# Attention value products in three 256-column chunks, two of them issued inside their own head

## The chip, the cores and the metric

The program runs on one core of a Trainium2 chip. The metric is the device time of one execution in microseconds (us), the median of the runs; lower is better.

## What is computed

The input holds queries, keys and values of 2 x 8 = 16 heads (here "heads" counts both batches), 768 rows of 64 channels each. Rows attend only inside their cluster; two mixture-of-experts layers follow, which the change doesn't touch.

```python
q_assign = argmax(einsum(q_n, c_n)); k_assign = argmax(einsum(k_n, c_n))
mask = q_assign[:, :, :, None] == k_assign[:, :, None, :]
scores = np.where(mask, scale * q @ k.T, -1e9)
attn = np.exp(scores - scores.max(-1)); attn /= attn.sum(-1) + 1e-9
return attn @ v                      # then _moe_ref and _moe2_ref
```

## The kernel before

All of the attention is one software pipeline over 16 heads `n`, each of six steps `t` of 128 query rows. The four compute engines and the DMA queue of SyncE (SP) each have their own program, written out by hand in `pair`, with counting semaphores between them; an engine works strictly in its own order. `j` is the parity of the head, `g = 6n + t`.

One step of 128 rows passes through these functions:

- **score** (TensorE, L1063 and L1064): two products of 512 and two of 256 columns into one of two score buffers. It is issued one step ahead.
- **row_top** (VectorE, L906): the maximum of the 768 scores of each row.
- **exp** (ScalarE, L731): the exponential, with the row's sum.
- **turn_probs** (TensorE, L1072): six 128x128 transposes, in two halves of three, into two PSUM banks (4 and 5). It is issued one step late.
- **high** (ScalarE, L714) copies the two halves, rounded to fp32r, into `p_hi`; **low** (VectorE, L912) writes the remainders into `p_lo`. The next `turn_probs` needs `low` of the same half.
- **sum_values** (TensorE, L1090 and L1091): the value product. For each of six key blocks it multiplies `v_both` (values, and their remainders in the other 64 columns) with `p_hi` and with `p_lo`, summed in the PSUM region `side` (banks 6 and 7). Part 0 and part 1 hold six products of 512 columns each, part 2 twelve of 256 columns.
- **o_copy** (ScalarE, L708) copies the sums to `o_sb`, first 512 columns, then 256. **fold_output** (TensorE, L1102, six matmuls recorded as twelve rows) turns them into rows and adds the two parts; **store_head** (VectorE, L932, L939, L946) scales and stores them.

For the head to come, TensorE computes cluster scores (**cluster_scores**, L1040), VectorE picks the cluster in five steps (**choose**, L881 to L897), TensorE turns the one-hot rows (**turn_onehot**, L1050), and ScalarE copies them into mask rows (**mask_rows**, L697 and L699). GpSimd splits queries and keys of a head (**split_qk**, L262 to L268) and its values (**split_v**, L596 and L599); SP loads them (**load_qk**, L473; **load_v**, L478).

TensorE's order in head `n` at each step is: score of `t+1`, turn_probs of `t-1`, and then

- t = 0: cluster scores of head n+1; t = 1: fold_output of head n-2; t = 2: turn_onehot of head n+1;
- t = 3, 4, 5: sum_values parts 0, 1, 2 of head **n-1**.

Part 0 waits until the mask rows are copied, since `side` overlaps the bank of the turned one-hot rows. ScalarE's order is: exp of `t`, high of `t-1`, and at t = 2 then mask_rows, at t = 5 then o_copy of the first 512 columns; the other 256 are copied at t = 0 of the next head. VectorE has store_head of head n-2 at t = 3. After the last head TensorE still has turn_probs, parts 0 and 1 of head 15, fold_output of head 14, part 2 and fold_output of head 15. `p_hi` and `p_lo` hold a whole head each, two buffers of each.

Of the kernel before, what the change touches and what calls it, by code (L numbers as in the profile page):

```python
# [14 lines left out]
F32 = mybir.dt.float32  # L15
# [7 lines left out]
P = 128  # L23
# [20 lines left out]
QK_SPLITS = 5  # L44
WIDE = DM + 2
# [13 lines left out]
def build(nc, q, k, v, centroids, w_gate, w_noise, noise, w1, w2, w_gate2, w1b, w2b, capacity, out):  # L59
# [6 lines left out]
    with ExitStack() as ctx:  # L66
# [14 lines left out]
        p_hi = [carve(QT * S).rearrange("p (k q) -> p k q", k=QT) for _ in range(2)]  # L81
        p_lo = [carve(QT * S).rearrange("p (k q) -> p k q", k=QT) for _ in range(2)]
# [88 lines left out]
        side = bank(6, 1024)  # L171
        o_sum = bank(7, QT * FOLD).rearrange("p (t d) -> p t d", t=QT)
        HALVES = ((0, 3), (3, 6))

        def turned_half(c):
            return bank(4 + c, 3 * P)

# [283 lines left out]
        def _(sp):  # L461
# [41 lines left out]
            with sp.Fori(1, HEADS // 2) as r:  # L503
                for j in range(2):
                    load_qk(2 * r + j, j)
                    load_v(2 * r + j - 1, 1 - j)

                blank(rows[0], TILES * DM, 4 * DM, r - 1)
# [44 lines left out]
        def _(gp):  # L553
# [37 lines left out]
            def split_v(m, j, r):  # L591

                gp.wait_ge(values_landed[j], 16 * (r + 1))
                need(gp, values_summed, 2 * (m - 1))
                gp.sem_inc(passed, 1)
                gp.tensor_copy(v_both[j][:, :, 0:D], v_raw[j]).then_inc(v_split, 1)  # L596
                gp.wait_ge(v_split, 2 * m + 1)
                gp.sem_inc(passed, 1)
                gp.tensor_tensor(v_both[j][:, :, D:P], v_raw[j], v_both[j].bitcast(F32)[:, :, 0:D],  # L599
                                 ALU.subtract).then_inc(v_split, 1)  # L600
# [86 lines left out]
        def _(act):  # L687
# [14 lines left out]
            def o_copy(n, part):  # L702

                act.wait_ge(values_summed, 2 * n + 1 + part)
                if part == 0:
                    need(act, o_folded, n)
                lo, hi = ((0, 512), (512, S))[part]
                act.activation(o_sb[:, lo:hi], side[:, lo:hi], ACT.Copy).then_inc(o_copied, 1)  # L708

            def high(g, j, t):  # L710

                for c, (a, b) in enumerate(HALVES):
                    act.wait_ge(probs_turned, 2 * g + c + 1)
                    act.activation(p_hi[j][:, a:b, t * P:(t + 1) * P],  # L714
                                   turned_half(c).rearrange("p (k q) -> p k q", k=3), ACT.Copy).then_inc(high_ready, 1)
# [4 lines left out]
            def pair(i, first=False, last=False):  # L720
                for j in range(2):
                    n = 2 * i + j
                    prepares = not (last and j == 1)
                    follows = not (first and j == 0)
                    for t in range(QT):
                        g = QT * n + t
                        act.wait_ge(top_ready, g + 1)
                        need(act, probs_turned, 2 * (g - 1))
                        if t == 0:
                            need(act, inv_step, 2 * (n - 1))  # L730
                        act.activation(probs[t % 2], scores[t % 2], ACT.Exp, bias=top[:, t % 2:t % 2 + 1],  # L731
                                       accum_out=sums[:, j, t:t + 1]).then_inc(probs_ready, 1)
                        if t == 0 and not first:
                            o_copy(n - 2, 1)
                        if t > 0:
                            if t == 1:
                                need(act, values_summed, 2 * (n - 1))
                            high(g - 1, j, t - 1)
                        elif follows:
                            high(g - 1, 1 - j, QT - 1)  # L740
                        if t == 2 and prepares:
                            mask_rows(n + 1, 1 - j, False)
                            mask_rows(n + 1, 1 - j, True)
                        if t == 5 and follows:
                            o_copy(n - 1, 0)
# [5 lines left out]
            high(QT * HEADS - 1, 1, QT - 1)  # L751
            o_copy(HEADS - 2, 1)
            o_copy(HEADS - 1, 0)
            o_copy(HEADS - 1, 1)

# [88 lines left out]
        def _(dve):  # L844
# [63 lines left out]
            def low(g, j, t, c):  # L908

                a, b = HALVES[c]  # L910
                dve.wait_ge(high_ready, 2 * g + c + 1)
                dve.tensor_tensor(p_lo[j][:, a:b, t * P:(t + 1) * P],  # L912
                                  turned_half(c).rearrange("p (k q) -> p k q", k=3),
                                  p_hi[j][:, a:b, t * P:(t + 1) * P].bitcast(F32), ALU.subtract).then_inc(low_ready, 1)
# [44 lines left out]
            def pair(i, first=False, last=False):  # L959
                for j in range(2):  # L960
# [3 lines left out]
                    for t in range(QT):  # L964
                        g = QT * n + t

                        def store_all():
                            if isinstance(i, int):
                                b, h = (n - 2) // H, (n - 2) % H
                            else:  # L970
                                b, h = bass.ds((i - 1) // 4, 1), bass.ds(2 * ((i - 1) % 4) + j, 1)
                            for step in range(3):
                                store_head(n - 2, j, b, h, step)
# [24 lines left out]
            dve.wait_ge(const_ready, 23)  # L998
# [7 lines left out]
            for j in range(2):  # L1006
                for step in range(3):
                    store_head(HEADS - 2 + j, j, B - 1, H - 2 + j, step)
# [20 lines left out]
        def _(pe):  # L1029
# [4 lines left out]
            def cluster_scores(m, j, r, h):  # L1034
# [3 lines left out]
                need(pe, o_copied, 2 * m - 5)  # L1038
# [37 lines left out]
            def sum_values(n, j, part, prepares=False):  # L1076


                if part == 0:
                    pe.wait_ge(low_ready, 2 * (QT * n + 4))  # L1080
                    pe.wait_ge(v_split, 2 * (n + 1))
                    need(pe, o_copied, 2 * n - 1)
                    if prepares:
                        pe.wait_ge(rows_ready, 2 * n + 6)
                if part == 2:
                    pe.wait_ge(low_ready, 2 * QT * (n + 1))
                    need(pe, head_stored, n)
                a, b = (512, S) if part == 2 else (0, 512)
                for kb in range(QT) if part == 2 else range(*HALVES[part]):
                    pe.matmul(side[:, a:b], v_both[j][:, kb, :], p_hi[j][:, kb, a:b], start=(kb == 0), stop=False)  # L1090
                    mm = pe.matmul(side[:, a:b], v_both[j][:, kb, :], p_lo[j][:, kb, a:b], start=False,  # L1091
                                   stop=(kb == QT - 1))
                if part:
                    mm.then_inc(values_summed, 1)

            def fold_output(n, h):


                pe.wait_ge(o_copied, 2 * n + 2)
                need(pe, head_stored, n)  # L1100
                for t in range(QT):
                    mm = pe.matmul(bank(7, 512)[:, t * FOLD:(t + 1) * FOLD + GROUP], o_sb[:, t * P:(t + 1) * P],  # L1102
# [8 lines left out]
            def pair(i, first=False, last=False):  # L1111
                for j in range(2):
# [3 lines left out]
                    for t in range(QT):  # L1116
# [12 lines left out]
                        if t == 1 and not first:  # L1129
                            fold_output(n - 2, 2 * ((i - 1) % 4) + j)  # L1130
                        if t >= 3 and follows:
                            sum_values(n - 1, 1 - j, t - 3, prepares)
                        if t == 2 and prepares:
                            turn_onehot(n + 1, 1 - j)

            pair(0, first=True)
            pe.wait_ge(const_ready, 23)
            pe.wait_ge(fold_landed, 64)
# [127 lines left out]
```

## Time and profile before

| | |
|---|---|
| median of 3 timed runs | 1020.16 us (1014.76, 1020.16 and 1021.29) |
| span of the profiled execution, first to last instruction | 1015.0 us |
| its own time beyond the span | not given |
| TensorE busy | 865.7 us (85%) |
| VectorE, ScalarE, GpSimd busy | 569.2, 349.7, 542.1 us |
| mean granted TensorE clock | 0.915 |

The profile is one execution. Each row names an engine (PE is TensorE's matmuls, PEld its weight loads, DVE VectorE, ACT ScalarE, POOL GpSimd), a source line and an operation. Attention takes the first 291 us or so. Ends of matmuls are modelled, so positions on TensorE are best read from starts.

### The profile page before, as it was taken

To read this page: it belongs to the slowest core of one execution; us is meant where nothing else is said; L and a number is where in the kernel's file an instruction comes from. 1 tells how busy PE (TensorE), PEld (TensorE's weight loads), DVE (VectorE), ACT (ScalarE), POOL (GpSimd) and SP (SyncE) were. 2 spreads that over 40 slices of the span, in tenths; PEclk is the share of its full clock that TensorE was granted. 3 is DMA by queue.
4 is the path that set the end of the run, shared out by engine and by line. 5 is a ranking of instruction groups with operands and counts; after the bars stand their busy time and mean duration, and the time that the engine had idled before them with its cause. 6 is when DMAs were issued, how large, how long until landed. Compare 5 with 4: busy or idle time off the path is not lost.

```text
span 1015.0 us, 16573 instructions
## 1 busy us (share of the span) xinstructions
PE 865.7 (85%) x4669; PEld 734.4 (72%) x4670; DVE 569.2 (56%) x907; ACT 349.7 (34%) x586; POOL 542.1 (53%) x338
## 2 busy tenths in 40 slices
PE   4899999999932199999999999999493099999995
PEld 3788888888832078888878887878393078888884
DVE  6888888888851044444444444444273436665552
ACT  3878787877840121131112212020000212343210
POOL 6666665657134863364334615160362926798563
PEclk9999999999975599999999999999755589999998
DMA  7544345346643653354334525251262624566422
GB/s 162 151 122 125 88 116 142 104 109 252 254 147 142 217 188 124 124 171 159 124 124 145 176 74 171 76 175 52 85 184 84 217 80 166 193 241 209 156 103 93
DMA packets 70742, 147.83 MB, mean 146 GB/s; under 512 B 23296, under 2 KB 23296, under 8 KB 68416
## 3 DMA queue, kind: packets, MB, share of 16 engines
q1 hardware_dynamic: 38096, 60.77, 19.8%
q10 hardware_dynamic: 26624, 67.12, 19.8%
q0 software_dynamic: 6000, 19.68, 5.7%
q8 instruction: 10, 0.16, 0.1%
q14 instruction: 12, 0.10, 0.0%
HBM read 107.66 MB, written 39.88 MB: 145 GB/s over the span
## 4 chain that ended last, share of the span: by engine, by line
PE 72%; issue 8%; POOL 7%; DVE 5%; DMA 3%; ACT 2%; SPq 1%; ACTq 0%; POOLq 0%; DVEq 0%
PE banks L1209 15%; PE banks L1211 15%; PE banks L1210 15%; PE banks L1072 5%; PE banks L1090 4%; POOL rows_by_slot L664 3%; PE banks L1091 3%; PE banks L1224 3%; PE banks L1063 3%; PE banks L1064 3%; PE banks L1040 2%; PE banks L1102 2%; PE banks L1200 2%; DMA tokens_and_shared<-rows_by_slot 2%; POOL tokens_and_shared L278 2%
## 5 line engine op out<-in xcount | busy, mean ns | idle before, releaser
L648 POOL TENSOR_TENSOR arena<-raw_ring,arena 128x1024 fp32r<-128x1024 f32 x128 | 302.3, 2399 | 262.5 <-ACT arena L786 262.1
L786 ACT ACTIVATE arena<-raw_ring 128x1024 fp32r<-128x1024 f32 x128 | 133.2, 1058 | 460.2 <-PE banks L1211 278.0
L1209 PE MATMUL banks<-arena,split_x 128*128 x352 | 143.0, 406 | 16.1 <-DVE split_x L416 14.4
L1209 PE MATMUL banks<-arena,split_h 128*128 x352 | 142.4, 405 | 7.5 <-DVE split_h L444 5.9
L1211 PE MATMUL banks<-arena,split_x 128*128 x352 | 139.8, 397 | 0.0
L1210 PE MATMUL banks<-arena,split_x 128*128 x352 | 139.5, 396 | 0.0
L1211 PE MATMUL banks<-arena,split_h 128*128 x352 | 138.6, 394 | 0.0
L1210 PE MATMUL banks<-arena,split_h 128*128 x352 | 138.4, 393 | 0.0
L422 DVE TENSOR_SCALAR tokens_and_shared<-banks 128x512 f32<-128x512 f32 x88 | 60.8, 690 | 104.5 <-PE banks L1211 104.0
L912 DVE TENSOR_TENSOR arena<-banks,arena 128x384 fp32r<-128x384 f32 x192 | 99.0, 542 | 19.5 <-ACT arena L714 19.5
L906 DVE TENSOR_REDUCE top<-banks 128x1 f32<-128x768 f32 x96 | 91.1, 949 | 21.4 <-PE banks L1064 20.6
L714 ACT ACTIVATE arena<-banks 128x384 fp32r<-128x384 f32 x192 | 85.0, 489 | 40.7 <-PE banks L1072 39.1
L731 ACT ACTIVATE tokens_and_shared<-banks,top 128x768 f32<-128x768 f32 x96 | 86.9, 905 | 15.2 <-DVE top L906 14.8
L1209 PEld LDWEIGHTS banks<-arena,split_x 128*128 128x128 f32 x352 | 67.4, 191 | 30.5 <-issue 17.4
L429 DVE COPY tokens_and_shared<-banks 128x512 f32<-128x512 f32 x29 | 20.1, 692 | 123.1 <-PE banks L1211 123.1
L1072 PE MATMUL banks<-ident,tokens_and_shared 128*128 128x128 f32 x576 | 84.9, 279 | 4.2 <-DVE arena L912 3.9
L1200 PE MATMUL banks<-ident,tokens_and_shared 128*128 128x128 f32 x184 | 28.7, 280 | 67.7 <-DMA tokens_and_shared<-rows_by_slot 67.7
L1209 PEld LDWEIGHTS banks<-arena,split_h 128*128 128x128 f32 x352 | 67.0, 190 | 21.5 <-issue 9.1
L1211 PEld LDWEIGHTS banks<-arena,split_x 128*128 128x128 f32 x352 | 67.2, 191 | 14.4
L1211 PEld LDWEIGHTS banks<-arena,split_h 128*128 128x128 f32 x352 | 66.9, 190 | 14.2
L1200 PEld LDWEIGHTS banks<-ident,tokens_and_shared 128*128 128x128 f32 x184 | 23.1, 143 | 74.7 <-DMA tokens_and_shared<-rows_by_slot 69.1
L1210 PEld LDWEIGHTS banks<-arena,split_x 128*128 128x128 f32 x352 | 67.5, 192 | 13.2
(161 smaller groups left out, 1466.9 us busy)
## 6 DMA issues: line engine op xcount, KB each, us to landing
raw_ring<-in_moe_w ACTq DMA_DIRECT2D x128, 512.0 KB, 3.4
rows_by_slot<-arena SPq DMA_DIRECT2D x8, 1024.0 KB, 6.0
raw_ring<-in_q SPq DMA_DIRECT2D x40, 192.0 KB, 3.5
raw_ring<-in_k SPq DMA_DIRECT2D x40, 192.0 KB, 4.0
tokens_and_shared<-rows_by_slot SPq DMA_DIRECT2D x30, 256.0 KB, 3.3
results_by_slot<-tokens_and_shared SPq DMA_DIRECT2D x29, 256.0 KB, 2.1
rows_by_slot<-arena SPq DMA_DIRECT2D x5, 1028.0 KB, 10.4
tokens_and_shared<-rows_by_slot SPq DMA_DIRECT2D x16, 257.0 KB, 3.7
```

The costliest lines, as they stand in the source:

```text
L422: dve.tensor_scalar(h_tile[:, half * 512:(half + 1) * 512], bank(2 + half, 512), 0.0, None, ALU.max).then_inc(z.relu_done, 1)
L648: gp.tensor_tensor(arena[:, lo:lo + PIECE], ring[:, slot * PIECE:(slot + 1) * PIECE], arena[:, hi:hi + PIECE].bitcast(F32), ALU.subtract). ...
L714: act.activation(p_hi[j][:, a:b, t * P:(t + 1) * P], turned_half(c).rearrange("p (k q) -> p k q", k=3), ACT.Copy).then_inc(high_ready, 1)
L731: act.activation(probs[t % 2], scores[t % 2], ACT.Exp, bias=top[:, t % 2:t % 2 + 1], accum_out=sums[:, j, t:t + 1]).then_inc(probs_ready, 1)
L786: act.activation(arena[:, hi:hi + PIECE], ring[:, slot * PIECE:(slot + 1) * PIECE], ACT.Copy).then_inc(w_high, 1)
L906: dve.tensor_reduce(top[:, b:b + 1], scores[b], AX, ALU.max, negate=True).then_inc(top_ready, 1)
L912: dve.tensor_tensor(p_lo[j][:, a:b, t * P:(t + 1) * P], turned_half(c).rearrange("p (k q) -> p k q", k=3), p_hi[j][:, a:b, t * P:(t + 1) * ...
L1072: mm = pe.transpose(turned_half(c)[:, (k - a) * P:(k - a + 1) * P], probs[t % 2][:, k * P:(k + 1) * P], ident[:, :])
L1200: mm = pe.transpose(bank(0, DM)[:, b * P:(b + 1) * P], x_tile[:, b * P:(b + 1) * P], ident[:, :])
L1209: pe.matmul(out_ap, left[:, 0, tile], hi, start=(b == 0), stop=False)
L1210: pe.matmul(out_ap, left[:, 0, tile], lo, start=False, stop=False)
L1211: mm = pe.matmul(out_ap, left[:, 1, tile], hi, start=False, stop=(b == blocks - 1))
```

## The change

`sum_values` now has three equal chunks of 256 columns, each of twelve products with its own sum in one PSUM region `summed` of 256 columns (bank 7). Chunks 0 and 1 of head n are issued in head n itself, at t = 4 and t = 5, chunk 2 at t = 1 of head n+1. fold_output moves to t = 3 and to head n-1, writes into bank 6 and waits for the mask rows; store_head moves to t = 4 and to head n-1. ScalarE copies chunk 0 at t = 5 after `high`, chunk 1 at t = 0 of the next head after `high`, chunk 2 at t = 2 before `mask_rows`. `p_hi` and `p_lo` shrink to two chunks each. GpSimd and SP take a head's values ahead of the next head's queries and keys. After the last head only chunk 2 and one fold_output are left.

```diff
-        p_hi = [carve(QT * S).rearrange("p (k q) -> p k q", k=QT) for _ in range(2)]
+        p_hi = [carve(QT * CHUNK).rearrange("p (k q) -> p k q", k=QT) for _ in range(2)]
...
-        side = bank(6, 1024)
-        o_sum = bank(7, QT * FOLD).rearrange("p (t d) -> p t d", t=QT)
+        summed = bank(7, CHUNK)
+        o_sum = bank(6, QT * FOLD).rearrange("p (t d) -> p t d", t=QT)
...
+            return (CHUNKS * j + t // 2) % 2, slice(t % 2 * P, (t % 2 + 1) * P)
...
+                    load_v(2 * r + j - 1, 1 - j)
                     load_qk(2 * r + j, j)
-                    load_v(2 * r + j - 1, 1 - j)
...
-                need(gp, values_summed, 2 * (m - 1))
+                need(gp, values_summed, CHUNKS * (m - 1))
...
+            split_v(0, 0, 0)
             split_qk(1, 1, 0)
-            split_v(0, 0, 0)
             with gp.Fori(1, HEADS // 2) as r:
+                split_v(2 * r - 1, 1, r - 1)
                 split_qk(2 * r, 0, r)
-                split_v(2 * r - 1, 1, r - 1)
+                split_v(2 * r, 0, r)
                 split_qk(2 * r + 1, 1, r)
-                split_v(2 * r, 0, r)
...
+            def high(g, n, j, t):
+
+                buf, at_q = chunk_place(j, t)
+                if t % 2 == 0:
+                    need(act, values_summed, CHUNKS * n + t // 2 - 1)
...
-                        if t == 0 and not first:
-                            o_copy(n - 2, 1)
                         if t > 0:
-                            if t == 1:
-                                need(act, values_summed, 2 * (n - 1))
-                            high(g - 1, j, t - 1)
+                            high(g - 1, n, j, t - 1)
                         elif follows:
-                            high(g - 1, 1 - j, QT - 1)
+                            high(g - 1, n - 1, 1 - j, QT - 1)
+                            o_copy(n - 1, 1)
+                        if t == 2 and follows:
+                            o_copy(n - 1, 2)
                         if t == 2 and prepares:
                             mask_rows(n + 1, 1 - j, False)
                             mask_rows(n + 1, 1 - j, True)
-                        if t == 5 and follows:
-                            o_copy(n - 1, 0)
+                        if t == 5:
+                            o_copy(n, 0)
...
-                            if t == 3 and not first and place == 2:
+                            if t == 4 and follows and place == 2:
...
+            def sum_values(n, j, chunk):
+
+
+                pe.wait_ge(low_ready, 2 * (QT * n + 2 * chunk + 2))
+                if chunk == 0:
                     pe.wait_ge(v_split, 2 * (n + 1))
...
+                need(pe, o_copied, CHUNKS * n + chunk)
+                buf = (CHUNKS * j + chunk) % 2
+                for kb in range(QT):
+                    pe.matmul(summed, v_both[j][:, kb, :], p_hi[buf][:, kb, :], start=(kb == 0), stop=False)
+                    mm = pe.matmul(summed, v_both[j][:, kb, :], p_lo[buf][:, kb, :], start=False,
                                    stop=(kb == QT - 1))
...
+                mm.then_inc(values_summed, 1)
+
+            def fold_output(n, h, turned):
+
+
+                pe.wait_ge(o_copied, CHUNKS * (n + 1))
+                pe.wait_ge(rows_ready, 2 * turned)
...
-                        if t == 1 and not first:
-                            fold_output(n - 2, 2 * ((i - 1) % 4) + j)
-                        if t >= 3 and follows:
-                            sum_values(n - 1, 1 - j, t - 3, prepares)
+                        if t == 1 and follows:
+                            sum_values(n - 1, 1 - j, 2)
                         if t == 2 and prepares:
                             turn_onehot(n + 1, 1 - j)
+                        if t == 3 and follows:
...
+                            fold_output(n - 1, 2 * ((i + j - 1) % 4) + 1 - j, n + 1 + prepares)
+                        if t >= 4:
+                            sum_values(n, j, t - 4)
...
             turn_probs(QT * HEADS - 1, QT - 1)
-            sum_values(HEADS - 1, 1, 0)
-            sum_values(HEADS - 1, 1, 1)
-            fold_output(HEADS - 2, H - 2)
             sum_values(HEADS - 1, 1, 2)
-            fold_output(HEADS - 1, H - 1)
+            fold_output(HEADS - 1, H - 1, HEADS)
```

## Rows read from the trace of the kernel before

**Rows 1.** Windows: each engine's busy time, clock, DMA share, GB/s, by stretch.

```profile
100.00:150.00 50.00, 49.72 (x347) 43.61 (x347) 43.14 (x86) 39.74 (x86) 31.79 (x22) 1.00 0.40 104
```

**Rows 2.** Waits between 50 and 250 us: total us, times, longest.

```profile
POOL arena L262 <- PE banks L1064: 64.2, 12, 5.4
...
PEld banks L1072 <- DVE arena L912: 4.2, 27, 0.2
PEld banks L1090 <- ACT arena L699: 3.9, 12, 0.4
```

**Rows 3.** Timeline of PE, head 5: start, duration, engine, line, operation.

```profile
104.07 0.82 PE L1072 MATMUL banks<-ident,tokens_and_shared 128*128 128x128 f32 x6
104.73 1.49 PE L1102 MATMUL banks<-fold_all,tokens_and_shared 128*128 x12
105.99 0.47 PE L1063 MATMUL banks<-arena 128*128 128x512 f32 x1
...
106.78 0.82 PE L1072 MATMUL banks<-ident,tokens_and_shared 128*128 128x128 f32 x6
...
109.88 0.50 PE L1090 MATMUL banks<-arena 128*128 128x512 f32 x1
...
111.37 0.40 PE L1063 MATMUL banks<-arena 128*128 128x512 f32 x1
...
112.08 0.82 PE L1072 MATMUL banks<-ident,tokens_and_shared 128*128 128x128 f32 x6
112.65 0.48 PE L1090 MATMUL banks<-arena 128*128 128x512 f32 x1
...
114.11 0.39 PE L1063 MATMUL banks<-arena 128*128 128x512 f32 x1
...
114.93 1.01 PE L1072 MATMUL banks<-ident,tokens_and_shared 128*128 128x128 f32 x6
115.70 0.36 PE L1090 MATMUL banks<-arena 128*128 128x256 f32 x1
...
117.20 0.40 PE L1063 MATMUL banks<-arena 128*128 128x512 f32 x1
```

**Rows 4.** Timeline of ACT in the same head.

```profile
107.31 0.87 ACT L714 ACTIVATE arena<-banks 128x384 fp32r<-128x384 f32 x2 [0.88 <-PE banks L1072]
108.20 0.80 ACT L697 ACTIVATE arena<-banks 16x768 fp32r<-16x768 bf16 x1
```

**Rows 5.** Lines by form, 50 to 250 us: busy, mean ns, idle before.

```profile
L714 ACT ACTIVATE arena<-banks 128x384 fp32r<-128x384 f32 x145 | 64.2, 489 | 27.5 <-PE banks L1072 26.1
...
L708 ACT ACTIVATE tokens_and_shared<-banks 128x256 f32<-128x256 f32 x12 | 4.7, 395 | 0.0
```

**Rows 6.** Timeline of PE: a step of heads 0, 1 and 14.

```profile
30.56 0.48 PE L1063 MATMUL banks<-arena 128*128 128x512 f32 x1
...
39.33 1.18 PE L1072 MATMUL banks<-ident,tokens_and_shared 128*128 128x128 f32 x6 [1.53 <-DVE arena L912]
...
255.93 0.82 PE L1072 MATMUL banks<-ident,tokens_and_shared 128*128 128x128 f32 x6
```

**Rows 7.** Windows in head 1, columns as in rows 1.

```profile
40.00:42.00 2.00, 2.00 (x11) 1.57 (x12) 1.97 (x4) 1.54 (x3) 0.99 (x1) 0.61 0.45 121
```

**Rows 8.** Timeline of PE in head 15 and after it.

```profile
268.78 0.98 PE L1072 MATMUL banks<-ident,tokens_and_shared 128*128 128x128 f32 x6 [0.41 <-DVE arena L912]
...
280.39 0.82 PE L1072 MATMUL banks<-ident,tokens_and_shared 128*128 128x128 f32 x6
...
286.26 0.36 PE L1090 MATMUL banks<-arena 128*128 128x256 f32 x1 [0.96 <-DVE tokens_and_shared L939]
...
288.41 1.59 PE L1102 MATMUL banks<-fold_all,tokens_and_shared 128*128 128x112 f32 x12 [0.47 <-ACT tokens_and_shared L708]
```

**Rows 9.** Timeline of DVE: the last `low`.

```profile
282.01 0.52 DVE L912 TENSOR_TENSOR arena<-banks,arena 128x384 fp32r<-128x384 f32 x1
```

**Rows 10.** Windows after the last head, columns as in rows 1.

```profile
284.00:286.00 2.00, 1.30 (x12) 1.12 (x11) 0.60 (x2) 0.60 (x1) 0.00 (x0) 1.00 0.00 0
```

More of the change, by code:

```diff
@@ L44 @@
 QK_SPLITS = 5
+CHUNK = 2 * P
+CHUNKS = S // CHUNK
 WIDE = DM + 2
@@ L79, in carve @@
             return arena[:, at[0] - size:at[0]]
-        p_hi = [carve(QT * S).rearrange("p (k q) -> p k q", k=QT) for _ in range(2)]
-        p_lo = [carve(QT * S).rearrange("p (k q) -> p k q", k=QT) for _ in range(2)]
+        p_hi = [carve(QT * CHUNK).rearrange("p (k q) -> p k q", k=QT) for _ in range(2)]
+        p_lo = [carve(QT * CHUNK).rearrange("p (k q) -> p k q", k=QT) for _ in range(2)]
         q_both, k_high, q_mask, k_mask = ([carve(S) for _ in range(2)] for _ in range(4))
@@ L176, in turned_half, with chunk_place @@
             return bank(4 + c, 3 * P)
+        def chunk_place(j, t):
+            return (CHUNKS * j + t // 2) % 2, slice(t % 2 * P, (t % 2 + 1) * P)
         passed = sem("passed")
@@ L700, in mask_rows, with o_copy @@
                                    scale=FAR, bias=-FAR).then_inc(rows_ready, 1)
-            def o_copy(n, part):
-                act.wait_ge(values_summed, 2 * n + 1 + part)
-                if part == 0:
+            def o_copy(n, chunk):
+                act.wait_ge(values_summed, CHUNKS * n + chunk + 1)
+                if chunk == 0:
                     need(act, o_folded, n)
-                lo, hi = ((0, 512), (512, S))[part]
-                act.activation(o_sb[:, lo:hi], side[:, lo:hi], ACT.Copy).then_inc(o_copied, 1)
-            def high(g, j, t):
+                act.activation(o_sb[:, chunk * CHUNK:(chunk + 1) * CHUNK], summed, ACT.Copy).then_inc(o_copied, 1)
+            def high(g, n, j, t):
+                buf, at_q = chunk_place(j, t)
+                if t % 2 == 0:
+                    need(act, values_summed, CHUNKS * n + t // 2 - 1)
                 for c, (a, b) in enumerate(HALVES):
                     act.wait_ge(probs_turned, 2 * g + c + 1)
-                    act.activation(p_hi[j][:, a:b, t * P:(t + 1) * P],
+                    act.activation(p_hi[buf][:, a:b, at_q],
                                    turned_half(c).rearrange("p (k q) -> p k q", k=3), ACT.Copy).then_inc(high_ready, 1)
@@ L750, in _ @@
             pair(HEADS // 2 - 1, last=True)
-            high(QT * HEADS - 1, 1, QT - 1)
-            o_copy(HEADS - 2, 1)
-            o_copy(HEADS - 1, 0)
+            high(QT * HEADS - 1, HEADS - 1, 1, QT - 1)
             o_copy(HEADS - 1, 1)
+            o_copy(HEADS - 1, 2)
             weights = ((w1, w2), (w1b, w2b))
@@ L910, in low @@
                 a, b = HALVES[c]
+                buf, at_q = chunk_place(j, t)
                 dve.wait_ge(high_ready, 2 * g + c + 1)
-                dve.tensor_tensor(p_lo[j][:, a:b, t * P:(t + 1) * P],
+                dve.tensor_tensor(p_lo[buf][:, a:b, at_q],
                                   turned_half(c).rearrange("p (k q) -> p k q", k=3),
-                                  p_hi[j][:, a:b, t * P:(t + 1) * P].bitcast(F32), ALU.subtract).then_inc(low_ready, 1)
+                                  p_hi[buf][:, a:b, at_q].bitcast(F32), ALU.subtract).then_inc(low_ready, 1)
             def invert(n, j, step):
@@ L968, in store_all @@
                             if isinstance(i, int):
-                                b, h = (n - 2) // H, (n - 2) % H
+                                b, h = (n - 1) // H, (n - 1) % H
                             else:
-                                b, h = bass.ds((i - 1) // 4, 1), bass.ds(2 * ((i - 1) % 4) + j, 1)
+                                b, h = bass.ds((i + j - 1) // 4, 1), bass.ds(2 * ((i + j - 1) % 4) + 1 - j, 1)
                             for step in range(3):
-                                store_head(n - 2, j, b, h, step)
+                                store_head(n - 1, 1 - j, b, h, step)
                         def between(place):
@@ L983, in between @@
                                 choose(n + 1, 1 - j, 2 + place)
-                            if t == 3 and not first and place == 2:
+                            if t == 4 and follows and place == 2:
+                                if first:
+                                    dve.wait_ge(const_ready, 23)
                                 store_all()
@@ L997, in _ @@
             pair(0, first=True)
-            dve.wait_ge(const_ready, 23)
             with dve.Fori(1, HEADS // 2 - 1) as i:
@@ L1005, in _ @@
             low(QT * HEADS - 1, 1, QT - 1, 1)
-            for j in range(2):
-                for step in range(3):
-                    store_head(HEADS - 2 + j, j, B - 1, H - 2 + j, step)
+            for step in range(3):
+                store_head(HEADS - 1, 1, B - 1, H - 1, step)
             for s in range(2):
@@ L1037, in cluster_scores @@
                 pe.wait_ge(head_landed[j], 16 * 6 * (r + 1))
-                need(pe, o_copied, 2 * m - 5)
+                need(pe, head_stored, m - 2)
                 for t in range(QT):
@@ L1074, in turn_probs @@
                     mm.then_inc(probs_turned, 1)
-            def sum_values(n, j, part, prepares=False):
-                if part == 0:
-                    pe.wait_ge(low_ready, 2 * (QT * n + 4))
+            def sum_values(n, j, chunk):
+                pe.wait_ge(low_ready, 2 * (QT * n + 2 * chunk + 2))
+                if chunk == 0:
                     pe.wait_ge(v_split, 2 * (n + 1))
[L1082 to L1091, printed above, removed]
-                                   stop=(kb == QT - 1))
[L1093 to L1100, printed above, removed]
+                need(pe, o_copied, CHUNKS * n + chunk)
[3 more added lines that the diff above has]
+                    mm = pe.matmul(summed, v_both[j][:, kb, :], p_lo[buf][:, kb, :], start=False,
+                                   stop=(kb == QT - 1))
+                mm.then_inc(values_summed, 1)
+            def fold_output(n, h, turned):
+                pe.wait_ge(o_copied, CHUNKS * (n + 1))
+                pe.wait_ge(rows_ready, 2 * turned)
                 for t in range(QT):
-                    mm = pe.matmul(bank(7, 512)[:, t * FOLD:(t + 1) * FOLD + GROUP], o_sb[:, t * P:(t + 1) * P],
+                    mm = pe.matmul(bank(6, 512)[:, t * FOLD:(t + 1) * FOLD + GROUP], o_sb[:, t * P:(t + 1) * P],
                                    fold_all[:, bass.ds(h * FOLD, FOLD + GROUP)], start=True, stop=True)
@@ L1128, in pair @@
                             cluster_scores(n + 1, 1 - j, i + j, 2 * ((i + j) % 4) + 1 - j)
-                        if t == 1 and not first:
-                            fold_output(n - 2, 2 * ((i - 1) % 4) + j)
-                        if t >= 3 and follows:
-                            sum_values(n - 1, 1 - j, t - 3, prepares)
+                        if t == 1 and follows:
+                            sum_values(n - 1, 1 - j, 2)
                         if t == 2 and prepares:
                             turn_onehot(n + 1, 1 - j)
+                        if t == 3 and follows:
+                            if first:
+                                pe.wait_ge(const_ready, 23)
+                                pe.wait_ge(fold_landed, 64)
+                            fold_output(n - 1, 2 * ((i + j - 1) % 4) + 1 - j, n + 1 + prepares)
+                        if t >= 4:
+                            sum_values(n, j, t - 4)
             pair(0, first=True)
-            pe.wait_ge(const_ready, 23)
-            pe.wait_ge(fold_landed, 64)
             with pe.Fori(1, HEADS // 2 - 1) as i:
```

## The prediction

> **What bounds the kernel now.** The page's busy times name TensorE first, but over stages with different limits, so I read the windows next. In the attention TensorE's matmuls fill 49.72 of 50 us at full clock, while VectorE has 43.14, ScalarE 39.74 and GpSimd 31.79 [rows 1]. The reader should see that TensorE is the bound there, and that VectorE and ScalarE have only some 15 to 20% of slack: a wait laid on TensorE is paid in full, and one laid on the others is paid soon. The view of waits gives what TensorE still waits for in 12 heads: 4.2 us for `low` before transposes (0.35 a head) and 3.9 us for the copy of the mask rows before part 0 (0.33 a head) [rows 2]. It also shows GpSimd waiting over 5 us in each head.
>
> The timeline gives the order and the price of each piece [rows 3]. `turn_probs` of step 1 starts at 106.78 in head 5 and at 255.93 in head 14 [rows 3, 6]: 149.15 us for 9 heads, 16.57 a head. From starts to starts, the prices I use are: transposes before fp32r products 0.57 (112.08 to 112.65), before fp32 ones 0.66 (104.07 to 104.73); fold_output 1.26 (104.73 to 105.99); six products of 512 columns 1.46 (112.65 to 114.11), 1.49 after a wait (109.88 to 111.37); twelve of 256 columns 1.50 (115.70 to 117.20), which I take as 1.53 after a wait; score 0.71 after fp32r products (111.37 to 112.08), 0.79 after fold_output (105.99 to 106.78). ScalarE's two `high` copies start 0.53 after the transposes and last 0.87, so they end 1.40 after them (107.31 and 106.78) [rows 3, 4].
>
> **The change in one middle head.** The work on TensorE hardly changes: 9216 columns of value product in 36 matmuls instead of 24. Twelve of 512 columns become 24 of 256: 1.50 in place of 1.46 for each of two parts. What changes is who waits for whom. I walk one head, with its `turn_probs` of step 1 at time 0.
>
> - *t = 2.* ScalarE ends `high` at 1.40. The copy of chunk 2 now stands ahead of the mask rows. A copy of 256 sums takes 0.395 [rows 5]; and a copy begins about 0.10 before the one ahead of it ends (two of 0.489 take 0.87 together) [rows 4, 5]. So the mask rows start at about 1.65 instead of 1.42 (108.20) and, with the 1.68 from there to the waiting matmul (109.88), TensorE goes on at 3.35 instead of 3.10: 0.25 late. It can be nothing, if ScalarE would have waited for the one-hot rows anyway, and 0.40, if nothing overlaps.
> - *t = 3.* What waits is now fold_output, at 1.26 + 0.03 instead of 1.49. score of step 5 starts at 4.64 (before: 111.37, which is 4.59).
> - *t = 4.* score 0.79, transposes at 5.43, chunk 0 at 6.00, next score at 7.50 (before 7.33). The exp of step 3 comes 0.25 late, so `low` of step 2 ends near 5.73, when the second half of these transposes (5.76) wants it: I count nothing, and at most 0.3. Queued behind them is all of TensorE.
> - *t = 5.* Transposes of step 4 at 8.21. store_head has left the place ahead of them on VectorE, so the 0.11 that score to transposes took longer there before (0.82 for 0.71) goes. Then chunk 1 needs `summed` empty, and there is one such region. Chunk 0 was finished before the transposes, but its copy stands behind `high` on ScalarE, and `high` needs these same transposes. So: `high` ends at 8.21 + 1.40 = 9.61, the copy starts at 9.51 and ends at 9.90, and TensorE goes on at 9.95, 1.74 after its transposes started, where before it took 0.77 (114.93 to 115.70). That is 0.97 more in each head, and it is the term that decides. With no overlap and a slower wake-up it is 1.94, and it can't fall under 1.69 while the order on ScalarE stands. Behind the waiting matmul on TensorE are chunk 1, the next score and everything else.
> - *t = 0 and 1.* Chunk 1 takes 1.53, score of the next head's step 1 at 11.48 (before 10.42). Chunk 1's copy is behind `high` again, but cluster_scores, a score and transposes lie between, so chunk 2 finds it done (copy ends near 13.9, chunk 2 wants to start at 15.5). Chunk 2 instead of fold_output: 0.57 + 1.50 + 0.71 = 2.78 for 2.71 (104.07 to 106.78).
>
> The next head's `turn_probs` of step 1 comes at 17.70: 1.13 us a head more than 16.57. The bounds of the pieces make this 0.9 to 1.8.
>
> **Costs at nothing, and their covers.** GpSimd's `split_v` now waits for the sums of the head two before, but falls in its wait of over 5 us for the last score [rows 2]; if that cover were gone, some 1.9 us would delay `split_qk`, which has several us until its score. SP's load of values ahead of queries adds one issue in front of six, and its condition is met a head earlier. store_head comes after `low` of step 3 and waits for a fold_output long done; it delays the row maximum of the next head's first step, whose exp is wanted only after the 0.97 wait. The half-size split buffers alternate: `high` of steps 0, 2 and 4 waits for the chunk two back, which TensorE has always issued before the transposes that `high` needs. One more ScalarE copy instruction a head costs about 0.2 us of an engine with 20% slack.
>
> **Start.** In head 0 the two chunks are new work where TensorE was not the bound. From the score at 30.56 [rows 6], where chunk 0 now stands: +1.50 score, +0.71 transposes, +1.74 chunk 1, +1.53 score, +0.71 transposes, +0.66 cluster scores, +1.26 score, +0.79 transposes, +0.57 chunk 2, +1.50 score, +0.71 gives 42.24 for `turn_probs` of step 1 in head 1, which came at 39.33 after 1.53 idle [rows 6]: 2.91 late. After that idle time the granted clock fell: 0.61 between 40 and 42 us [rows 7]. From 39.33 to 106.78 were 67.45 us instead of 4 x 16.57 = 66.28, so one such fall costs about 1.2. Chunk 2 fills this hole, and I take the fall as gone (if not, 1.2 more).
>
> **Middle.** Heads 1 to 14 are 13 periods: 13 x 17.70 = 230.1 instead of 216.6 (39.33 to 255.93), 13.5 more. From there to head 15's first transposes 1.06 more (all but the 0.07 of t = 1).
>
> **Tail.** Before, from the transposes at 268.78 to fold_output of head 15 at 288.41 are 19.63 us [rows 8]. After: 0.77 + 1.50 + 0.71 + 0.57 + 1.02 (score with a wait for `low`) + 0.75 + 1.26 + 0.79 + 0.57 + 1.50 to the transposes of step 4; + 1.74 + 1.53 to those of step 5; then `low` of them (282.01 + 0.52 against transposes at 280.39: 2.14) [rows 8, 9] and 0.12 to wake; then 2.15 from the last chunk to fold_output (286.26 to 288.41). Together 17.12: 2.5 less. Parts 0 and 1, a fold_output and the 0.96 wait between them are gone from there.
>
> **Sum.** 2.91 + 13.5 + 1.06 - 2.5 = 15.0 us later at the end of the attention. The layers after it are chained behind it and not touched. On the profile that is 1015.0 to 1030.0 us of span; its own time beyond the span isn't given, and the span lies at the low end of the timed runs. I put the difference on their median: 1020.2 + 15.0 = 1035.2 us, 1.5% more.
>
> **Rivals.**
>
> A. *The copy is not late* (the other side). The place is ScalarE's queue at t = 5, the price 1.17 a head. If the copy of chunk 0 were done when the transposes are (0.57 after their start), a head would take 16.53, the start would be 1.74 late, the tail 3.7 shorter, and the total would be 1.74 - 13 x 0.04 - 0.1 - 3.7 = -2.6: 1017.6, not slower. If the wait for mask rows also vanished (0.33 [rows 2] in 14 heads), it would be 1013. For it: ScalarE has slack, and chunk 0 is finished early. Against: an engine works in order, and `high` can't end before 1.40. It decides where the copy ends under 0.6 after the transposes start.
>
> B. *TensorE's clock falls in the new wait.* Each head would have a hole of 1.2 us, and a hole of 1.53 cost 1.2 us in head 1 [rows 6, 7]. In 15 heads this is 18 more: 1053. Against: in the wait of 0.96 before 286.26 [rows 8] the clock stayed at 1.00 [rows 10], and the middle stays about 93% busy. The Trainium skill (TensorE: Matmul & The Clock Gate, "A second HAM failure mode: psum-queue depth-cycling") warns of just this pattern: short idle times between groups of matmuls that take turns in PSUM can make the clock swing. By that rule the sum would be 1053; this trace has no case of a periodic hole to confirm it.
>
> C. *More waits come up.* VectorE's `low` of step 2 is 0.03 before its limit at t = 4 by my walk, and store_head stands before the row maximum at t = 5. With 0.4 more in each of 14 heads: 1041. For it: VectorE is 86% busy. Against: the old waits for `low` came where store_head stood, and it has moved to where TensorE waits anyway.
>
> **How the numbers follow.** Forecast 0.78, A 0.12, B 0.04, C 0.06. About 1% is what a measurement tells from no change; it is 10.2 us here. The forecast's own spread (0.9 to 1.8 a head, 2 us for start and tail) is +10 to +27 with most of it near 15, so 0.07 of it falls within 1%; of A, 0.04 is faster by over 1% (if other waits go as well and the runs lie low) and 0.08 within. Faster 0.04, same 0.15, slower 0.81. The range of 1024 to 1046 takes in nearly all of the forecast's spread and C, and below it part of the way to A; it leaves out A and B.
>
> **What would show it.** Right: among the waits a new one of the first product's weight load on the ScalarE copy of the sums, once a head and about 1.2 us each; a period of 17.7 us; chunk 2 in the hole of head 1 at full clock; the last fold_output near 303 instead of 288.41. Wrong: a period under 17.0; clock under 1.00 between 50 and 280 us; a large wait for VectorE at t = 4 or 5.

## The result, and the profile after

The changed kernel took 1042.03 us (median of 4 runs, 1040.93 to 1043.76) against 1018.88 us before: a ratio of 1.0248, with a 95% interval of 1.0213 to 1.0284. It is slower, by 23 us where 15 were forecast. The profiled execution took 1041.61 us with a span of 1039.9 us, 24.9 us over the span before.

The page's head line and busy times of the changed kernel (columns: busy us, share of the span, instructions):

```profile
span 1039.9 us, 17028 instructions
...
PE 870.0 (84%) x4861; PEld 742.5 (71%) x4862; DVE 572.0 (55%) x907; ACT 351.1 (34%) x602; POOL 544.3 (52%) x338
```

There are 192 more matmuls (16 heads x 12) and hardly any more work: TensorE is busy 870.0 us instead of 865.7. So 20.6 of the 24.9 us are idle time of TensorE (169.9 us outside its busy time for 149.3). The windows say where (the row that answers to [rows 1]):

```profile
100.00:150.00 50.00, 45.34 (x341) 40.72 (x340) 38.38 (x73) 35.77 (x79) 30.19 (x19) 1.00 0.37 105
```

TensorE has 45.34 of 50 us instead of 49.72, at full clock. The layers behind the attention are the same: VectorE's first instruction of the routing comes at 317.68 instead of 292.92, 24.76 later, which is all of the difference but 0.1.

The waits between 60 and 260 us, 11 heads, name one that TensorE did not have before and one that has grown (total us, times, longest):

```profile
PEld banks L1092 <- ACT tokens_and_shared L713: 12.6, 11, 1.1
...
PE banks L1103 <- ACT arena L705: 6.8, 11, 0.7
...
PEld banks L1079 <- DVE arena L919: 4.3, 21, 0.2
```

The first is chunk 1 waiting for the copy of chunk 0, 1.15 us a head. The second is the wait for the mask rows, now 0.62 a head at fold_output instead of 0.33 at part 0 [rows 2]. The third, for `low` before the transposes, is as large as before. The timeline of TensorE over one head shows the positions (start, duration; the rows that answer to [rows 3]; line numbers have moved: score L1070, transposes L1079, products L1092, fold_output L1103):

```profile
109.32 0.40 PE L1070 MATMUL banks<-arena 128*128 128x512 f32 x1
...
110.03 0.82 PE L1079 MATMUL banks<-ident,tokens_and_shared 128*128 128x128 f32 x6
...
112.81 1.07 PE L1079 MATMUL banks<-ident,tokens_and_shared 128*128 128x128 f32 x6
113.64 0.36 PE L1092 MATMUL banks<-arena 128*128 128x256 f32 x1
...
115.15 0.40 PE L1070 MATMUL banks<-arena 128*128 128x512 f32 x1
...
115.87 0.99 PE L1079 MATMUL banks<-ident,tokens_and_shared 128*128 128x128 f32 x6
...
119.45 1.59 PE L1103 MATMUL banks<-fold_all,tokens_and_shared 128*128 x12 [0.53 <-ACT arena L705]
120.81 0.48 PE L1070 MATMUL banks<-arena 128*128 128x512 f32 x1
...
124.40 0.82 PE L1079 MATMUL banks<-ident,tokens_and_shared 128*128 128x128 f32 x6
126.13 0.39 PE L1092 MATMUL banks<-arena 128*128 128x256 f32 x1 [0.91 <-ACT tokens_and_shared L713]
```

From the transposes at 124.40 to chunk 1 at 126.13 are 1.73 us. ScalarE's timeline shows what chunk 1 waits for:

```profile
124.93 0.87 ACT L722 ACTIVATE arena<-banks 128x384 fp32r<-128x384 f32 x2 [1.04 <-PE banks L1079]
125.68 0.39 ACT L713 ACTIVATE tokens_and_shared<-banks 128x256 f32<-128x256 f32 x1
```

L722 is `high`, which starts 0.53 after the transposes that it needs; L713 is the copy of chunk 0, behind it in the queue, and it ends at 126.07. In the mean of 12 heads it is 1.73 us too.

And from the transposes at 112.81 to chunk 2 at 113.64 are 0.83, where an undisturbed hand-over takes 0.57. The period of a head, taken from one copy of the mask rows to the next, is 18.39 us (from 44.09 in head 1 to 283.16 in head 14, 13 periods); in the kernel before it is 16.62 in the same way (41.33 to 257.36). What delays chunk 2 stands in the timelines of VectorE and GpSimd:

```profile
111.11 1.19 DVE L927 TENSOR_SCALAR inv<-sums 128x6 f32<-128x6 f32 x1
112.21 0.54 DVE L919 TENSOR_TENSOR arena<-banks,arena 128x384 fp32r<-128x384 f32 x1
...
112.77 0.51 DVE L919 TENSOR_TENSOR arena<-banks,arena 128x384 fp32r<-128x384 f32 x1
```

```profile
110.45 1.81 POOL L272 TENSOR_TENSOR arena<-raw_ring,arena 64x768 fp32r<-64x768 f32 x1 [0.18 <-POOL arena L270]
```

The reader should see the ends: `invert`, six numbers a partition, takes 1.19 us and ends at 112.30; GpSimd's product, which began before it, ends at 112.26. The lines by source give the same for 13 heads: 1034 ns at least, 1156 in the middle. In each of the 13 it ended 0.02 to 0.04 us after GpSimd's product did. Behind the last head GpSimd has nothing left to do, and there the instruction is short:

```profile
295.02 0.16 DVE L927 TENSOR_SCALAR inv<-sums 128x6 f32<-128x6 f32 x1
```

Before the change it took 160 ns in the middle of 14 heads, since it fell between two of GpSimd's products. `low` of step 5 stands behind it, and the transposes behind `low`.

### The profile page after: what moved, and what is told of

Same layout as the page of the kernel before. It is cut to its first block, busy times and chain, and to the rows that moved or that the text cites. A ratio compares the mean times of both kernels' runs of the same rounds, so it can differ in the third digit from the quotient of the medians.

```text
span 1039.9 us, 17028 instructions
## 1 busy us (share of the span) xinstructions
PE 870.0 (84%) x4861; PEld 742.5 (71%) x4862; DVE 572.0 (55%) x907; ACT 351.1 (34%) x602; POOL 544.3 (52%) x338
## 4 chain that ended last, share of the span: by engine, by line
PE 49%; POOL 8%; issue 7%; DVE 3%; DMA 2%; ACT 0%; SPq 0%; POOLq 0%; DVEq 0%
PE banks L1210 15%; PE banks L1212 14%; PE banks L1211 14%; POOL rows_by_slot L670 3%; PE banks L1225 3%; POOL tokens_and_shared L284 2%; PE banks L1201 2%; DMA tokens_and_shared<-rows_by_slot 1%; POOL out_rows L688 1%; POOL arena L654 1%; DVE tokens_and_shared L419 1%; PE banks L1187 0%; DMA rows_by_slot<-tokens_and_shared,slot_i 0%; DVE tokens_and_shared L318 0%; DVE tokens_and_shared L330 0%
## 5 line engine op out<-in xcount | busy, mean ns | idle before, releaser
L722 ACT ACTIVATE arena<-banks 128x384 fp32r<-128x384 f32 x192 | 86.6, 489 | 73.1 <-PE banks L1079 72.2
L1092 PE MATMUL banks<-arena 128*128 128x256 f32 x288 | 75.0, 296 | 16.6 <-ACT tokens_and_shared L713 15.2
L1079 PE MATMUL banks<-ident,tokens_and_shared 128*128 128x128 f32 x576 | 85.7, 278 | 1.5 <-ACT tokens_and_shared L739 0.8
```

The lines of the kernel that those rows point to most:

```text
L722: act.activation(p_hi[buf][:, a:b, at_q], turned_half(c).rearrange("p (k q) -> p k q", k=3), ACT.Copy).then_inc(high_ready, 1)
L1079: mm = pe.transpose(turned_half(c)[:, (k - a) * P:(k - a + 1) * P], probs[t % 2][:, k * P:(k + 1) * P], ident[:, :])
L1092: pe.matmul(summed, v_both[j][:, kb, :], p_hi[buf][:, kb, :], start=(kb == 0), stop=False)
```

## The experiments

All are the changed kernel with one edit, but for one on the kernel before. The total time scatters by several us in the layers behind the attention. Their part is 722 us of the two spans above and 723 to 727 in six of the profiled executions below; it is 740 and 743 in the two that ran on a chip where the kernel before is 14 us slower too (1033.55 us). So each run is also read by its period of a head. Each period comes from one execution, but kernels that should have the same one agree within 0.05 us (18.39 and 18.44, 16.54 and 16.54), which is small beside the differences below.

**The copy of chunk 0 ahead of `high`.**

```diff
+                        if t == 5:
+                            o_copy(n, 0)
                         if t > 0:
                             high(g - 1, n, j, t - 1)
...
-                        if t == 5:
-                            o_copy(n, 0)
```

> The changed kernel, but ScalarE copies chunk 0 ahead of the two high copies at t = 5 instead of behind them. Theory (the copy behind high is what TensorE waits for, 1.16 us a head): chunk 1 starts 0.57 us after its transposes, and 16 heads x 1.16 = 18.6 us go; if VectorE's invert then falls out of GpSimd's product as well, up to 0.35 more a head, so 1042.0 becomes 1018 to 1024. Rival (VectorE and ScalarE are so near their bound that another wait takes its place): less than 6 us go, over 1036.

1022.16 us (10 runs), a ratio of 1.0022 to before (0.9997 to 1.0047): 20 us are gone, as the theory has it. The period fell by 1.57, to 16.82. TensorE in this run:

```profile
116.63 0.82 PE L1079 MATMUL banks<-ident,tokens_and_shared 128*128 128x128 f32 x6
117.21 0.36 PE L1092 MATMUL banks<-arena 128*128 128x256 f32 x1
```

From transposes to chunk 1 are 0.58 instead of 1.73: 1.15 of the 1.57. ScalarE does the same work; it has only stopped putting `high` ahead of a copy whose input was ready. Of the other 0.42, the timeline of VectorE shows where it went:

```profile
120.50 0.31 DVE L927 TENSOR_SCALAR inv<-sums 128x6 f32<-128x6 f32 x1
```

With the head shorter, `invert` meets only the end of one of GpSimd's products (118.96 + 1.82 = 120.78, and `invert` ends at 120.81).

**`invert` at t = 2.**

```diff
-                            if t == 0 and follows and place < 2:
+                            if t == 2 and follows and place < 2:
                                 invert(n - 1, 1 - j, place)
```

> The changed kernel, but VectorE issues the two invert instructions at t = 2 instead of t = 0. Theory (invert waits about 1 us for GpSimd's tensor_tensor to end, low of step 5 is late behind it, and TensorE's chunk 2 0.35 us late): 14 heads x 0.35 = 5 us go, 1037. Rival (invert's duration is covered, since low waits for high anyway): 1042.

1040.89 us (4 runs, 1038.01 to 1042.98). By the total it would be a miss. The period says otherwise: 17.98, 0.41 less, a little over the 0.35 of the theory, and in TensorE's timeline chunk 2 follows its transposes after 0.57:

```profile
113.11 0.82 PE L1079 MATMUL banks<-ident,tokens_and_shared 128*128 128x128 f32 x6
113.68 0.36 PE L1092 MATMUL banks<-arena 128*128 128x256 f32 x1
```

The attention ended at 313.91 instead of 317.68. It did not keep all of 13 x 0.41 = 5.3, since the copy of the mask rows in head 1 came at 45.59 instead of 44.09 (1.5 us later; those copied in head 0, where this edit changes nothing, were already 1.7 us late, so this is scatter of the start); and the layers behind it took 3 us more in this execution. So the mechanism is shown by the period and the rows, and the total is too coarse for it.

**The copy of chunk 2 ahead of `high`.**

```diff
+                        if t == 2 and follows:
+                            o_copy(n - 1, 2)
                         if t > 0:
                             high(g - 1, n, j, t - 1)
...
-                        if t == 2 and follows:
-                            o_copy(n - 1, 2)
```

> The changed kernel, but ScalarE copies chunk 2 at t = 2 ahead of the two high copies, not between them and the mask rows. Theory (the copy pushes the mask rows, and fold_output waits for these): 15 heads x 0.3 = 4 us go, 1038. Rival (the mask rows are held by the one-hot transposes, or the copy only moves the delay into high): 1042 or more.

1041.39 us (4 runs, 1038.53 to 1047.72), again too coarse. The period is 18.13, 0.26 less, near the 0.3 expected, and the attention ends at 315.05. TensorE's wait for the mask rows fell from 6.8 us in 11 heads to:

```profile
PE banks L1103 <- ACT arena L705: 3.9, 11, 0.4
```

**All three.**

> The changed kernel with all three edits: copy of chunk 0 ahead of high, copy of chunk 2 ahead of high, invert at t = 2. Theory (three separate waits of TensorE, 1.16 + 0.35 + 0.3 us a head): 25 to 28 us go, 1014 to 1017, faster than the kernel before (1018.9) because the tail is shorter. Rival (they overlap, or TensorE meets VectorE's bound): no less than 1022.

1015.21 us (5 runs), a ratio of 0.9949 (0.9904 to 0.9993). The period is 16.54; the three single edits add up to 1.57 + 0.41 + 0.26 = 2.24, but only 1.85 went. The missing 0.39 is `invert`, counted twice: the early copy of chunk 0 had already taken it out of GpSimd's product. The total lies in the theory's 1014 to 1017, but the theory of three separate waits that add up is wrong; the next run tests this.

**Both copies early, `invert` where it was.**

> The changed kernel with the copies of chunk 0 and of chunk 2 ahead of high, invert left at t = 0. Theory (once the copy of chunk 0 is early, the head is short again and invert falls between two of GpSimd's products, so moving it adds nothing): the same period as with all three edits, 16.54 us a head, and 1015 us. Rival (invert still costs 0.35 a head): 16.9 us a head, 1020.

The period is 16.54 again, and the attention ends at 291.52 (291.78 with all three). So `invert` costs TensorE nothing once the head is short, although it still takes 0.31 us in the middle of 13 heads. The total was 1031.54 us, on a chip where the kernel before took 1033.55 in the same series: 0.9986 (0.9954 to 1.0018). The 1020 of the rival and the 1015 of the theory can't be told apart by this total; the rival's period of 16.9 is out.

**The copy of chunk 0 still later.**

```diff
-                        if t == 5:
+                        if last and j == 1 and t == 5:
                             o_copy(n, 0)
...
                         elif follows:
+                            o_copy(n - 1, 0)
                             high(g - 1, n - 1, 1 - j, QT - 1)
```

> The changed kernel, but ScalarE copies chunk 0 still later, behind the exp of the next head's step 0 (in the last head where it was). Theory (TensorE pays this copy's lateness in full): the copy starts some 1.07 us later in 15 heads, 16 us more, 1056 to 1060, a period of 19.4 to 19.5 us. Rival (the price of the wait is shared with other slack on TensorE, so that a second microsecond costs less): under 1050.

1092.65 us (2 runs) against 1033.55 before on that chip, a ratio of 1.058; the period is 20.45. Both theories missed: 1.07 a head more was expected over 18.39, and 2.06 came. TensorE shows what was left out:

```profile
114.58 0.82 PE L1080 MATMUL banks<-ident,tokens_and_shared 128*128 128x128 f32 x6
117.25 0.39 PE L1093 MATMUL banks<-arena 128*128 128x256 f32 x1 [1.85 <-ACT tokens_and_shared L713]
117.48 0.28 PE L1094 MATMUL banks<-arena 128*128 128x256 f32 x1
...
117.89 0.42 PE L1093 MATMUL banks<-arena 128*128 128x256 f32 x1
118.10 0.41 PE L1094 MATMUL banks<-arena 128*128 128x256 f32 x1
...
119.60 0.63 PE L1071 MATMUL banks<-arena 128*128 128x512 f32 x1
...
120.88 0.96 PE L1080 MATMUL banks<-ident,tokens_and_shared 128*128 128x128 f32 x6
121.67 1.50 PE L1048 MATMUL banks<-tokens_and_shared,raw_ring 128*128 x12
```

The wait grew by 0.94 in the head shown (2.67 from the transposes instead of 1.73). And after it the products take 0.21 each instead of 0.12: the clock has fallen. Chunk 1 takes 2.35 (117.25 to 119.60) for 1.54 in the changed kernel, the score 1.28 for 0.71 and the transposes 0.79 for 0.66: 1.5 us in a head. The windows of that stretch (the clock is the third column from the end):

```profile
116.00:118.00 2.00, 0.75 (x5) 0.75 (x6) 0.67 (x2) 1.20 (x3) 1.72 (x2) 0.94 0.00 0
118.00:120.00 2.00, 2.00 (x10) 1.93 (x10) 0.00 (x0) 0.00 (x0) 1.82 (x2) 0.50 0.00 0
120.00:122.00 2.00, 2.00 (x13) 1.88 (x12) 0.88 (x2) 0.46 (x2) 1.66 (x2) 0.71 0.00 0
122.00:124.00 2.00, 2.00 (x18) 1.91 (x17) 1.87 (x7) 1.57 (x5) 0.00 (x0) 1.00 0.00 0
```

0.50 is the lower of the two levels, 1.2 GHz. Wait and clock together are more than the 2.06, since about 0.45 came back at the same time: in this longer head `invert` falls behind GpSimd's products, takes 0.16 in all 13 heads, and chunk 2 follows its transposes after 0.57 again. Over 50 to 250 us the granted clock is 0.90 to 0.93 in each 50 us, where it is 1.00 in the changed kernel. This is rival B of the prediction, one step further along.

**The old order on GpSimd and SP.**

```diff
-            split_v(0, 0, 0)
             split_qk(1, 1, 0)
+            split_v(0, 0, 0)
             with gp.Fori(1, HEADS // 2) as r:
-                split_v(2 * r - 1, 1, r - 1)
                 split_qk(2 * r, 0, r)
+                split_v(2 * r - 1, 1, r - 1)
...
```

> The changed kernel with the old order on GpSimd and SP (queries and keys ahead of values). Theory (GpSimd's split of the values is covered in either place, and the start of split_qk hangs on the last score of a head in both): within 3 us of 1042.0. Rival (the new order is what puts GpSimd's products beside VectorE's invert): 5 us or more faster.

1043.68 us (4 runs), a period of 18.44 instead of 18.39, and `invert` still takes 1145 ns in the middle: no change. The order of the splits is free in either place, and it is not what brought GpSimd's product beside `invert`.

**The kernel before, in products of 256 columns.**

```diff
-                a, b = (512, S) if part == 2 else (0, 512)
-                for kb in range(QT) if part == 2 else range(*HALVES[part]):
+                a, b = 256 * part, 256 * part + 256
+                for kb in range(QT):
```

> The kernel before, with its three parts of the value product as three times twelve products of 256 columns, at the same places (t = 3, 4, 5) and with the same waits, copies and buffers. Theory (twelve of 256 columns take 1.50 us, six of 512 take 1.46): 16 x 2 x 0.04 = 1.3 us slower than before. Rival (the smaller products cost some 0.03 us each in issue): 24 x 16 x 0.03 = 11 us slower.

1021.54 us (12 runs), a ratio of 1.0015 (0.9999 to 1.0032) to before, 1.5 us by the ratio and 3.3 at most; the period went from 16.62 to 16.69. The theory's 1.3 us fits, the 11 us of the rival are out. Smaller products are not what the change pays for.

A second region for the sums, so that chunk 1 need not wait at all, was not tried: scores, transposes, one-hot rows and the folded output take the other seven PSUM banks (the scores leave half of two of them free), and a region in such a half or in the other half of bank 7 would have one engine read a bank while TensorE writes it. No run here shows what that does.

## Why the prediction was right, and what it sized wrong

- *The term that decides.* Predicted 1.74 us from the transposes of step 4 to chunk 1; measured 1.73. The early copy brings it to 0.58 and takes 20 us off the total. Right, and shown: the copy ends 1.67 after the transposes (126.07), where the walk had 1.69 (9.90 for 8.21).
- *The start.* `turn_probs` of step 1 in head 1 was put at 42.24; it came at 42.26. Chunk 2 filled the hole there, and the clock stayed up (compare [rows 7]; in the changed kernel chunk 2 starts at 40.05):

```profile
40.00:42.00 2.00, 2.00 (x17) 1.94 (x16) 2.00 (x5) 1.63 (x3) 0.11 (x1) 1.00 0.39 74
```

- *The tail.* Predicted 2.5 us shorter. Measured from head 15's first transposes to the last fold_output:

```profile
295.79 0.99 PE L1079 MATMUL banks<-ident,tokens_and_shared 128*128 128x128 f32 x6 [0.32 <-DVE arena L919]
...
313.17 1.59 PE L1103 MATMUL banks<-fold_all,tokens_and_shared 128*128 128x112 f32 x12 [0.47 <-ACT tokens_and_shared L713]
```

17.38 instead of 19.63 [rows 8]: 2.25 shorter. Right. (The 303 that the prediction named for this instruction became 313, with the period.)

- *The period.* Predicted 17.70, measured 18.39. In 13 periods the missing 0.69 makes 9.0 of the 9.9 us by which the sum fell short. This is the part that was sized wrong: 1.13 more a head was forecast, and 1.8 came. Two terms make up nearly all of it. The step "t = 0 and 1" counted 0.57 + 1.50 + 0.71 after the transposes of step 0 and took `low` of step 5 as ready; it was late behind `invert`, held by GpSimd, and this part of the head is 0.34 longer in the head shown (score to transposes 0.87 for 0.79, then 0.83 for 0.57), 0.31 in the mean of 12 heads. The step "t = 2" put fold_output at 3.35; it came at 3.58 (115.87 to 119.45), and at 3.66 in the mean: 0.12 because the transposes there waited on VectorE and `high` took 0.99 for 0.87, the rest because no overlap came between the copy and the mask rows (117.28 + 0.38, then 117.68) and because 1.77 for 1.68 passed from the mask rows to the waiting matmul. (The sum itself was loose there: by its own prices the mask rows start at 1.60, not 1.65, and 1.65 + 1.68 is 3.33.) The remaining 0.07 is mostly fold_output, which took 1.34 in the mean for the 1.29 allowed. Moving `invert` gave back 0.41, since it also ended VectorE's delay of the transposes at t = 2; moving the copy of chunk 2 gave 0.26.
- *Why that was missed.* The prediction listed covers for GpSimd's own delay, but never asked what a longer head does to the overlap of GpSimd with VectorE. GpSimd's split starts with a score of one head and runs for 9.4 us before and 9.6 after the change, whatever TensorE does; a wait put into the head moves VectorE's t = 0 against it. The Trainium skill (SBUF — State Buffer, "Terms") says that VectorE and GpSimd share a pair of ports and that the one that comes second is blocked until the other's instruction ends. This trace agrees: 112.30 against 112.26 above. One pair of the kernel before does not fit: a VectorE addition of 128x96 (L946) at 112.83, beside GpSimd's scaling of the queries (112.53 to 114.74), took 0.72 us for the 0.27 it takes after the change, and yet ended at 113.55, well before GpSimd. It was slowed, but not held to the end.
- *Costs at nothing.* Order on GpSimd and SP: no cost found. Smaller products, priced at 1.3 us: 1.5, somewhere from 0 to 3.3. store_head at t = 4: no wait of TensorE behind it in the table of waits.
- *Rivals.* A, that the copy is not late, is out as a description of the change; but its total is what the early copy makes of it (1022 against the 1018 it named). B did not happen at a hole of 0.91 to 1.06 us idle, and did at 1.85 to 1.96, where it cost 1.5 us a head for the 1.2 that it named. C was right in kind: more waits came up, 0.69 a head, but at t = 1 and t = 2 and not where it put them.
- *What the change can give.* With the copies early, the period is that of the kernel before (16.54 against 16.62; without head 1, where the clock fell before, it is 16.55 against 16.57), the tail is 3.5 us shorter (32.1 from the last copy of mask rows to the routing, for 35.6), and the start gives 3.3 of it back (44.63 against 41.33 for those copied in head 1). Of these 3.3, 2.1 were already there at the mask rows copied in head 0 (28.23 against 26.12), before the first chunk is issued; that point lies anywhere from 25.93 to 28.23 in these runs, and no trace says why. So the attention ends 1.1 to 1.4 us earlier in the two executions, 0.1% of the run, and some 3 us would be an estimate for starts that are alike. The 0.5% measured for it on one chip and the 0.1% on another are the only totals; that more than the 1.1 us comes from it is not shown.

## What to carry to other kernels

When one PSUM region takes several sums in turn, its copy is on TensorE's path: put it ahead of any work of the copying engine that itself waits for a later instruction of TensorE. A wait added to a pipeline is not paid once: it shifts engines against each other, so walk the period again and look for VectorE instructions that come to lie beside long GpSimd ones. And read small edits by the period in the trace where the rest of the program scatters by more than they are worth.

## What the runs showed of the hardware that was not expected

With chunk 0 copied still later, TensorE's clock fell in every head to its lower level after an idle time of 1.85 to 1.96 us in 20, and cost 1.5 us a head beyond the wait (the three groups of matmuls behind it, timed above), while idle times of 0.91 to 1.06 us in 18.4 left it at 1.00 throughout. A single hole of 1.53 us in the kernel before [rows 6, 7] was followed by a fall too. The Trainium skill (TensorE: Matmul & The Clock Gate, "HAM oscillation — how this bites in real kernels") speaks of longer holes than these; here the clock fell after shorter ones.

A VectorE instruction of six numbers a partition took 1.16 us instead of 0.16, seven times as long, for no reason in itself or in its inputs, but for what GpSimd was doing: in 13 of 13 heads it ended within 0.04 us of the end of GpSimd's product, and with GpSimd idle it took 0.16.
